# Experts' transposes moved from TensorE to VectorE: 32-column blocks, quarter gathers, a store and fetch of the hidden rows, and the second product two tiles behind

## What is computed

```
logits = x @ w_gate ;  e = argmax, or the expert of the token before   # 8 experts
h = maximum(x[b, s] @ w1[e], 0.0)        # 512 -> 1024
out[b, s] = p[e] * (h @ w2[e])           # 1024 -> 512
```

## Time and profile before

| | us |
|---|---|
| median of 3 runs | 492.14 (491.46 to 493.25) |
| the profiled execution, own time | 491.42 |
| its span, first to last instruction | 489.6 |
| TensorE busy | 458.9 |
| VectorE busy | 262.9 |
| ScalarE busy | 221.5 |
| GpSimd busy | 194.0 |

### The profile page before, as it was taken

One profiled execution on the slowest core, in us unless ns is written; L12 is line 12 of the kernel. 1 busy time (PEld: TensorE's weight loads), 2 busy tenths in 40 slices (PEclk: granted clock), 3 DMA queues, 4 the chain that ended last, 5 costly groups with the idle time before them and its releaser, 6 DMA issues.

```text
span 489.6 us, 12908 instructions
## 1 busy us (share of the span) xinstructions
PE 458.9 (94%) x4154; PEld 368.7 (75%) x4155; DVE 262.9 (54%) x419; ACT 221.5 (45%) x393; POOL 194.0 (40%) x248
## 2 busy tenths in 40 slices
PE   8999999998998388999999999999999999999981
PEld 4888888886776255788888888888888888888860
DVE  5678888886666876335255252525527373522220
ACT  3777787777573031425345332524527272411110
POOL 7777877878690011122222222422223424132200
PEclk9999999998999569999999999999999999999996
DMA  8989999997045595133624513461564646021000
GB/s 178 189 193 186 187 191 201 202 217 200 2 118 139 131 343 61 27 138 122 212 84 175 195 43 93 161 198 53 205 212 177 222 192 207 37 75 30 29 27 6
DMA packets 86560, 69.22 MB, mean 141 GB/s; under 512 B 47998, under 2 KB 71038, under 8 KB 86528
## 3 DMA queue, kind: packets, MB, share of 16 engines
q1 hardware_dynamic: 82032, 57.78, 44.5%
q0 software_dynamic: 4496, 11.03, 7.4%
HBM read 59.34 MB, written 10.76 MB: 143 GB/s over the span
## 4 chain that ended last, share of the span: by engine, by line
PE 86%; DVE 5%; SPq 3%; issue 2%; ACT 1%; POOL 1%; DMA 1%; POOLq 0%; DVEq 0%; ACTq 0%
PE psum L1458 53%; PE psum L1476 4%; PE psum L1194 4%; PE psum L1176 3%; PE psum L1267 3%; PE psum L1282 2%; PE psum L1436 2%; PE psum L1230 2%; PE psum L1360 2%; PE psum L1204 2%; PE psum L1296 2%; PE psum L1370 2%; PE psum L1253 1%; PE psum L1243 1%; PE psum L1378 1%
## 5 line engine op out<-in xcount | busy, mean ns | idle before, releaser
L1458 PE MATMUL psum<-w_ring,xg_t 128*128 x552 | 133.9, 398 | 2.3 <-DVE xg_t L1115 1.6
L1458 PE MATMUL psum<-w_ring,h_t 128*128 x552 | 134.3, 398 | 1.7 <-issue 1.7
L1458 PEld LDWEIGHTS psum<-w_ring,xg_t 128*128 128x128 f32 x552 | 102.2, 188 | 25.0 <-issue 2.7
L1458 PEld LDWEIGHTS psum<-w_ring,h_t 128*128 128x128 f32 x552 | 101.9, 188 | 24.7 <-issue 2.0
L633 POOL DMA_INDIRECT out<-tile_bufs,to_row x23 | 23.5, 1023 | 191.9 <-DVE tile_bufs L1130 191.9
L1103 DVE TENSOR_TENSOR w_ring<-w_ring (+1 forms) x28 | 63.0, 2290 | 27.2 <-ACT w_ring L783 27.2
L783 ACT CAST w_ring<-w_ring (+1 forms) x28 | 52.1, 1908 | 34.6 <-DMA w_ring<-moe_w 34.6
L804 ACT ACTIVATE tile_bufs<-psum 128x512 f32<-128x512 f32 x46 | 25.0, 596 | 86.5 <-PE psum L1458 86.5
L1115 DVE TENSOR_TENSOR xg_t<-psum,xg_t 128x512 fp32r<-128x512 f32 x24 | 16.5, 690 | 83.2 <-ACT xg_t L797 83.2
L811 ACT CAST h_t<-psum 128x512 fp32r<-128x512 f32 x46 | 24.7, 591 | 74.2 <-PE psum L1476 74.2
L1130 DVE TENSOR_SCALAR tile_bufs<-psum,slot_w 128x512 f32<-128x512 f32 x23 | 17.2, 749 | 56.5 <-PE psum L1458 51.6
(11 more groups left out here) (181 smaller groups left out, 624.2 us busy)
## 6 DMA issues: line engine op xcount, KB each, us to landing
w_ring<-moe_w SPq DMA_DIRECT2D x15, 2048.0 KB, 8.8
early<-q SPq DMA_DIRECT2D x32, 144.0 KB, 3.9
early<-k SPq DMA_DIRECT2D x32, 144.0 KB, 3.8
early<-v SPq DMA_DIRECT2D x16, 288.0 KB
x_rows<-early SPq DMA_DIRECT2D x48, 96.0 KB, 2.5
early<-v SPq DMA_DIRECT2D x32, 120.0 KB
w_ring<-moe_w SPq DMA_DIRECT2D x8, 256.0 KB, 6.0
early<-v SPq DMA_DIRECT2D x64, 13.5 KB
```

The lines of the kernel that those rows point to most:

```text
L1458: ins = mm(bank[b][:, :], rows, w_ring[:, bass.ds(at + (off + c * width + n * 512), 512)], start=(c == 0 and k == 0), stop=(c == chunks - ...
```

## The change

TensorE's transposes in the expert part go, except for tile 0. VectorE transposes blocks of 32x32 within each group of 32 partitions instead. Such a transpose does not move data from one group of 32 partitions (a quadrant) to another, so the rows are brought to their quadrants by DMA:

- For x: the columns of `x_rows` are stored in four quarters, and each tile is gathered in four indirect DMAs of 128 columns each, where the partition picks both the token and the quarter (`from_part`). VectorE then transposes 512 columns into `x_raw` (`x_tr`).
- For h: ScalarE stores each relu half to a DRAM tensor `h_rows`, waits for the store, and fetches it back in four DMAs into `h_part`, each 32 partitions by four pieces of 256 columns (`h_back`). VectorE then transposes two halves of 512 columns into `h_raw` (`h_tr`).

`xg_t` and `h_t` get a second buffer each. The second product is two tiles behind the first. The halves of the w1 split stand on either side of `h_hi`, and the w2 split comes two tiles behind. Tile 0 is put in place by 16 matmuls with the identity (`first_x`). The gate weights are loaded in eight DMAs in place of two, in the new column order; VectorE computes `from_part` in 16 small instructions.

```diff
@@ gpsimd
             def gather(t):
                 wait(pool, s_xgt, t - 1)
-                pool.indirect_dma_start(xg[:, t % 2, :], None, x_rows[:, :],
-                                        bass.IndirectOffsetOnAxis(from_row[:, t:t + 1], 0),
-                                        bounds_check=NTOK - 1, oob_is_err=False).then_inc(s_xg[t % 2], 16)
+                for s in range(QUADS):
+                    if t == 1:
+                        pool.wait_ge(s_from, QUADS * (s + 1))
+                    pool.indirect_dma_start(xg[:, t % 2, s * 128:(s + 1) * 128], None, x_parts[:, :],
+                                            bass.IndirectOffsetOnAxis(from_part[:, t, s:s + 1], 0),
+                                            bounds_check=QUADS * NTOK - 1, oob_is_err=False).then_inc(s_xg[t % 2], 16)
...
+                if t >= 6:
+                    scatter(t - 6)
+                if t >= 4:
+                    gather_w(t - 4)
@@ scalar
+            def relu(t):
+                wait(act, s_h, t + 1)
+                wait(act, s_ht, 2 * t)
                 for n in range(2):
-                    wait(act, s_h, t + 1)
-                    if n == 0:
-                        wait(act, s_ht, 2 * t)
-                    nc.scalar.activation(h_act[:, n * 512:(n + 1) * 512], bank[1 + n][:, :], ACT.Relu).then_inc(s_relu, 1)
+                    cols = slice(n * 512, (n + 1) * 512)
+                    nc.scalar.activation(
+                        h_act[:, cols].rearrange("p (a c j) -> p a c j", a=2, j=32),
+                        psum[:, 1:3, :].rearrange("p b (c a j) -> p a (b c) j", a=QUADS, j=32)[:, 2 * n:2 * n + 2],
+                        ACT.Relu).then_inc(s_relu, 1)
+                    wait(act, s_relu, 2 * t + n + 1)
+                    act.dma_start(h_rows[:, cols], h_act[:, cols]).then_inc(s_hw[n], 16)
+
+            def h_back(t):
+                for a in range(QUADS):
+                    wait(act, s_hw[a // 2], 16 * (t + 1))
+                    act.dma_start(h_part[32 * a:32 * a + 32, :].rearrange("p (s n) -> p s n", s=QUADS),
+                                  h_rows.rearrange("(s i) (a n) -> a i s n", s=QUADS, a=QUADS)[a]).then_inc(s_hp, 16)
...
+            def tile(t, par, x=True, w=True):
                 relu(t)
-                if more:
-                    xgt_hi(t + 1)
-                split_next_hi(t - 1, s_w2_in, s_w2_hi, W1C, W2C)
+                if x:
+                    x_hi(t + 2, par)
+                h_back(t)
+                if w:
+                    split_next_hi(t, s_w1_in, s_w1_hi, 0, W1C, 0, 1)
+                h_hi(t, par)
+                if w:
+                    split_next_hi(t, s_w1_in, s_w1_hi, 0, W1C, 1, 2)
+                split_next_hi(t - 2, s_w2_in, s_w2_hi, W1C, W2C, 0, 2)
@@ vector
+            def x_tr(t, par, came):
+
+                wait(dve, s_xg[par], 64 * came)
+                wait(dve, s_xgt_out, t)
+                V.transpose(x_raw[:].rearrange("p (g s i) -> p s g i", s=QUADS, i=32),
+                            xg[:, par, :].rearrange("p (s g j) -> p s g j", s=QUADS, j=32)).then_inc(s_xgt, 1)
...
+            def h_tr(t):
+                wait(dve, s_hp, 16 * QUADS * (t + 1))
+                wait(dve, s_ht_out, 2 * t)
+                parts = h_part[:].rearrange("p (s c j) -> p s c j", s=QUADS, j=32)
+                for n in range(2):
+                    V.transpose(h_raw[:, n * 512:(n + 1) * 512].rearrange("p (c s i) -> p s c i", s=QUADS, i=32),
+                                parts[:, :, 4 * n:4 * n + 4, :]).then_inc(s_ht, 1)
...
+                if x:
+                    x_tr(t + 2, par, half + 2 + par)
+                    x_lo(t + 2, par)
+                h_tr(t)
+                h_lo(t, par)
+                y_scale(t - 2, par, half)
+                if w:
                     split_next_lo(t, s_w1_hi, s_w1, 0, W1C)
-                    xgt_lo(t + 1)
-                split_next_lo(t - 1, s_w2_hi, s_w2, W1C, W2C)
-                y_scale(t - 1, par, half)
@@ tensor
             def two_tiles(m):
 
-                w = first_product(2 * m, weights_of(2 * m), ahead=2 * m - 1)
-                x_transposes(2 * m + 1, 1, m)
-                w = second_product(2 * m - 1, 1, w, ahead=2 * m + 1)
-                h_transposes(2 * m)
-                w = first_product(2 * m + 1, w, ahead=2 * m)
-                x_transposes(2 * m + 2, 0, m + 1)
-                second_product(2 * m, 0, w)
-                h_transposes(2 * m + 1)
+                w = first_product(2 * m, 0, weights_of(2 * m), ahead=2 * m - 2)
+                w = second_product(2 * m - 2, 0, w, ahead=2 * m + 1)
+                w = first_product(2 * m + 1, 1, w, ahead=2 * m - 1)
+                second_product(2 * m - 1, 1, w)
```

More of the change, by code:

```diff
@@ L57, in build @@
     HP = NHEAD // 2
+    QUADS = 4
+    assert HP * 2 * HD == D and 2 * HD == 32 * QUADS
     VDMA = 8
@@ L1429, in _, with first_x @@
             keep_warm(WARM_TILES, 7)
-            def x_transposes(t, par, half):
-                wait(pe, s_xg[par], 16 * (half + 1))
-                wait(pe, s_xgt_out, t)
-                for c in range(KD):
-                    last = nc.tensor.transpose(bank[0][:, c * 128:(c + 1) * 128], xg[:, par, c * 128:(c + 1) * 128],
-                                               ident[:])
+            def first_x():
+                pe.wait_ge(s_x0, 16)
+                for g in range(KD):
+                    for a in range(QUADS):
+                        last = mm(bank[0][32 * a:32 * a + 32, g * 128:(g + 1) * 128],
+                                  xg[:, 0, a * 128 + g * 32:a * 128 + (g + 1) * 32], ident[:], start=True, stop=True)
                 last.then_inc(s_xgt, 1)
@@ L1443, in weights_of, with products @@
                         pe.value_load(tab_w[0:1, one(t)], min_val=0, max_val=PLACE))
-            def products(banks, rows_t, chunks, at, width, ahead):
+            def products(banks, rows_t, chunks, at, width, ahead, s_half=None, half=None):
                 for c in range(chunks):
@@ L1482, in second_product @@
                 pe.wait_ge(s_w2, e * PIECES + PIECES)
-                wait(pe, s_ht_out, 2 * t + 2)
+                wait(pe, s_ht_out, 2 * t + 1)
                 wait(pe, s_y_out, t - 1)
-                last, next_one = products((5 + par,), h_t, KF, at + W1C, D, ahead)
+                last, next_one = products((5 + par,), h_t[:, par], KF, at + W1C, D, ahead, s_ht_out, 2 * t + 2)
                 last.then_inc(s_y, 1)
```

232 lines of the change are left out of this document (124 added, 108 removed).

## The result

The changed kernel takes **574.69 us** (median of 4 executions, 572.22 to 576.91). The kernel before, on the same chip, takes 491.80 (4 executions, 490.09 to 493.25). The ratio is 1.1686, 95% interval 1.1621 to 1.1750: slower by 17%. I had forecast 526 us and a range to 562, so the direction was right and the size was outside the range.

The account below looks back on a forecast made before the run. TensorE bounded the kernel; after the change ScalarE's relu-to-relu time would. Relu(2) at 221.1 + 20 x 11.2 + 6 x 8.6 = 496.7, last second product from 507.7, 16.45 to the end, 1.8 around the span: 526 us, range 490 to 562.

Parts of the forecast that it names:

- The 0.7 us by which the profiled run lay under the median: End of the sum: the profiled run before the change was 0.7 us under its median, set beside the 526 us total.
- Either could be 0 to 4 us; I take 1 for both: At each of 6 expert changes: VectorE finishing behind ScalarE's casts, and h transfers sharing DMA engines with loads; 1 us together.
- The rest of the sum: Expert part: 11.2 us from relu to relu, plus weight casts and table reads of 7.6 us at each expert change.
- TensorE's tile: Expert part: without transposes TensorE's tile is two products, 5.58 + 5.59 = 11.17 us, instead of 12.48.
- The idle time in front of the first product: Sign in the expert tiles: TensorE idle before the first product's matmuls, released by ScalarE's relu; no size given.
- The start: Tiles 0 to 2: first product from about 190.3 us, ending at 196, relu(1) at 206.3, relu(2) at 221.1.
- The 1.8 us that I had added for the 16 matmuls: Tile 0: first_x has 16 matmuls where four transposes took 0.60 us, adding at least 1.8 us.
- Costed at nothing: Work taken to stay off the path: GpSimd's gathers, VectorE's work, gate loads, from_part, the later w2 load; 0 us.
- The waits of the load of w1(6) behind w2(5): SyncE's queue: w1(6) leaves 5.6 us late, relu some 7 us late at TensorE's pace; mostly waited out at ScalarE's.
- Landings at their long end: Rival, 13%: DMA landings of 3.5 and 3.8 us make 13.0 us from relu to relu in plain tiles; total 562 us.
- The clock falls: Rival, 6%: TensorE's clock drops to 1.2 GHz in the waits; were it so in five tiles, 566 us.
- The round trips fit: Rival, 15%: h's DRAM round trips fit, relu to relu below 9.5 us, so TensorE binds again; 472 us.

Follow-up runs that it names:

- fetch_last: The changed kernel with h cast and transposed one tile later, fetches issued behind the weight casts and first weights released earlier: 484.94 us, ratio 0.9803 to the kernel before.
- plain_fetch: The changed kernel with the four fetches of h replaced by one in plain rows of 4 KB (second product of wrong numbers): 554.33 us, one execution.

## Why the prediction was wrong in size

**Where the 49 us went** (574.69 against 526; of these 46.3 lie in the traced span, 570.5, forecast 524.2). Relu(2) came at 227.4, forecast 221.1: +6.3. The 20 laps took 316.7, forecast 20 x 11.2 + 6 x 8.6 = 275.6: +41.1. From relu(22) to the end 26.4, forecast 27.5: -1.1. The 0.7 us by which the profiled run lay under the median is named in the forecast's sum and not added.

**The step that failed** is the sentence "Either could be 0 to 4 us; I take 1 for both" on what an expert change adds besides its casts. The landings beside the loads cost 9.1 us at each change (574.69 - 520.08, over 6). The lag of VectorE behind the casts is the smaller term: without loads, in the six laps behind a w1 split, the fetches go out 4.0 to 4.8 us after the store, in the others from relu(1) on 2.1 to 3.1, since the cast of x ahead of them waits for VectorE. I had read slot_w's 2.5 us without a load and 6.6 beside one, and took a quarter of that difference, once. The round trip has two landings in series; 2 x 4.1 = 8.2 was in the rows. I had also placed only w1's load beside the lap. w2's came in the same lap at four of the changes: at 252.42 and 262.67 in the lap shown, where each of the two landings met a load of its own, and within 1.1 us of each other at relu(14) and relu(16). Two loads cost a lap 10.3 to 11.0 us, one 4.2 to 5.9.

**The rest of the sum held.** Without loads the 20 laps take 264.1 us; the forecast without its 6 us for this term is 20 x 11.2 + 6 x 7.6 = 269.6. The four laps there without a split in them or just before them are 10.8, 11.9, 10.9 and 11.1, forecast 11.2. Part of that is luck, since within the lap errors cancelled:

```profile
L848 ACTq DMA_DIRECT2D h_rows<-tile_bufs x46: 332/345/357, 201.4 to 545.7; - x46
...
L853 ACTq DMA_DIRECT2D h_part<-h_rows x92: 309/442/1368, 207.5 to 548.3; - x92
```

A fetch's issue took 0.44 us (median), not 0.61, and a store's 0.345, not 0.37. From the beginning of the last fetch's issue to VectorE's transpose it is 3.0 to 3.8 in laps without a load (5.2 in one), where I had 2.5. The transpose takes 0.69 (0.65), the cast 0.62 (0.59).

**TensorE's tile** of 11.17 us is right: 11.1 in the run where nothing else binds. The idle time in front of the first product, released by relu L843, and a ScalarE list full of waits for h_raw are there as forecast.

**The start** was forecast 6.3 us too early. The first product began at 192.34 (190.3 forecast), held by a release that stands behind VectorE's row numbers, a wait that I hadn't walked; it then took 8.39 us instead of 5.86, at a granted clock of 0.67, a mean of its two levels (1.2 and 2.4 GHz), behind 5.5 us without work; and the first fetch went out 6.1 us after its store, where ordinary laps have 2.0 to 3.7. The 1.8 us that I had added for the 16 matmuls were 0.5.

**Costed at nothing.** GpSimd's DMAs stayed off the path. The waits of the load of w1(6) behind w2(5) were, as forecast, waited out: the two are issued at 413.8 and 414.8. But there they make one burst of 4 MB beside relu(14), a lap of 23.3.

**The rivals.** *Landings at their long end* comes closest by its number (562), and its reason, traffic beside the loads, is the right one; it spread the cost over all laps, where it lies in six. *The clock falls* is there (granted clock 0.86 in the loaded lap, 1.00 in the ordinary ones, rows above; 0.77 over the first product of that lap), but that product, 7.34 us long, ends at 262.65, as the landed stores let the fetches go, and the relu that needs it comes 13.5 us later. Of the two slow products shown here, only tile 0's is on the path. *The round trips fit* would have needed laps of 9.5 us. Something like it comes true when the round trip is taken off ScalarE's path, by the edits of fetch_last: 485 us.

## What to carry to other kernels

Before a DMA round trip is put on a path, list the large loads that run in the same stretch, and price each landing in series beside them by a row that was measured beside such a load, not by the quiet one. If the trip can't be kept out of the way of loads, give its consumer a whole tile of slack and issue it behind all work that doesn't need it: those two edits, with the earlier release at the start, took this kernel from 575 to 485 us, under the 491 of before. Cutting the loads into pieces with a pause between them moved the wait to the weights instead. And count packets, not bytes alone: beside the load a fetch in pieces of 1 KB had a fifth of the load's bytes, a fetch in rows of 4 KB three quarters (0.52 MB to 0.68, from 268.7 to 271.9 us in plain_fetch).

## What the runs showed that I had not expected

- A small transfer on ScalarE's queue is held up by a 2 MB load on SyncE's. From the issue of the last 128 KB fetch to VectorE's transpose it is 4.2 to 10.7 us beside a load and 3.0 to 3.8 without (5.2 in one lap); for fetches of 16 KB 8.4 in the lap shown, and 1.7 to 2.3 without a load. The cost goes with the load's size (loaded laps 75.9, 102.0 and 128.0 us for 32 KB, 1 MB and 2 MB) and doesn't grow with the number of fetches (129.4 with eight, 128.0 with four).
- Beside each other the two queues moved about as many packets (493 and 421 in 7 us), whatever the packets held, so 512 packets of 1 KB ended together with the load's 512 of 4 KB. The run with an eighth of h's bytes and the run with eight fetches both left the 512 packets as they were.
- VectorE's 32x32 block transpose of 128x512 float32 takes 0.69 us into a contiguous buffer (h) and 0.71 for x, about as long as a subtraction of that size (0.69).
- The 16 matmuls with the identity, which stand in the trace as 32 records, took 1.08 us, where four full transposes took 0.60; I had added 1.8.
- The store after the first relu lands late even without a weight load: its last packet moved 9.5 us after its issue with the earlier release (205.3) and 5.9 without (207.3), where the 4.5 KB stores to `w_rows` and a gather are late as well. What slows them isn't shown.
